# Two buffers each for K and V of a head pair, with their loads requested one job ahead, in a fused attention and two-MLP kernel

## The reference

```python
# q, k, v: (2 batches, 8 heads, 768 positions, 64)
k_sum = k.reshape(B, H, nb, block, D).max(axis=3)       # block 32, nb 24
v_sum = v.reshape(B, H, nb, block, D).mean(axis=3)
scores_l = scale * q @ k.T          # kept where |i - j| < 16, else -1e9
scores_s = scale * q @ k_sum.T + log(block)
a = softmax(concat(scores_l, scores_s)); out = a @ concat(v, v_sum)
x = out as (1536 tokens, 512)
h = relu(x @ w_in);  x = (h * h) @ w_out                 # 512 -> 2048 -> 512
h = x @ w2_in;  solu = h * softmax(h)                    # 512 -> 1024
out = (layer_norm(solu) * g_ln) @ w2_out                 # 1024 -> 512
```

## Time and profile before

| | |
|---|---|
| median of three runs | 531.06 us (530.66 to 531.28) |
| span of the profiled execution | 529.4 us (no separate time was kept for it) |
| TensorE matmul busy | 492.2 us, 93% of the span |
| TensorE weight loads busy | 436.5 us, 82% |
| VectorE busy | 268.0 us, 51% |
| ScalarE busy | 223.8 us, 42% |
| GpSimd busy | 36.2 us, 7% |
| read from and written to HBM | 40.08 MB and 9.44 MB |
| mean granted TensorE clock | 0.970 |

### The profile page before, as it was taken

One profiled execution on the slowest core, in us unless ns is written; L12 is line 12 of the kernel. 1 busy time (PEld: TensorE's weight loads), 2 busy tenths in 40 slices (PEclk: granted clock), 3 DMA queues, 4 the chain that ended last, 5 costly groups with the idle time before them and its releaser, 6 DMA issues.

```text
span 529.4 us, 8722 instructions
## 1 busy us (share of the span) xinstructions
PE 492.2 (93%) x3088; PEld 436.5 (82%) x3088; DVE 268.0 (51%) x548; ACT 223.8 (42%) x553; POOL 36.2 (7%) x45
## 2 busy tenths in 40 slices
PE   3346699999999999999999999999999999999997
PEld 2235499999989999989999999999987888888875
DVE  5456276576575455564644454355374444444330
ACT  3345366556464444453443443333243233333331
POOL 0005411211100000000000000000010000000000
PEclk9966599999999999999999999999999999999999
DMA  7367453342450311232210034222062112211011
GB/s 228 114 207 273 140 156 87 120 140 79 138 181 36 95 36 64 87 133 93 79 40 1 1 104 165 69 61 59 21 195 64 60 62 79 78 60 59 22 39 40
DMA packets 29783, 49.82 MB, mean 94 GB/s; under 512 B 2272, under 2 KB 16864, under 8 KB 29248
## 3 DMA queue, kind: packets, MB, share of 16 engines
q1 hardware_dynamic: 23424, 30.65, 18.9%
q10 hardware_dynamic: 4608, 8.39, 5.4%
q0 software_dynamic: 1728, 10.49, 5.3%
HBM read 40.08 MB, written 9.44 MB: 94 GB/s over the span
## 4 chain that ended last, share of the span: by engine, by line
PE 91%; issue 4%; DVE 2%; DMA 1%; ACT 0%; SPq 0%; ACTq 0%
PE bank L790 27%; PE bank L765 26%; PE bank L896 13%; PE bank L917 13%; PE bank L726 5%; PE bank L746 3%; PE bank L735 2%; PE bank L908 2%; DMA v_raw<-vT 1%; DMA q_sb<-qT 0%; DVE k_ext L535 0%; PE bank L754 0%; DVE k_sum L540 0%; DVE neg_max L557 0%; DVE probs L553 0%
## 5 line engine op out<-in xcount | busy, mean ns | idle before, releaser
L790 PE MATMUL bank<-h_hi,wout_hi 128*128 128x384 f32 x256 | 91.1, 356 | 0.4 <-DVE h_lo L610 0.4
L765 PE MATMUL bank<-x_hi,win_hi 128*128 (+1 forms) x256 | 90.2, 352 | 0.8 <-DVE x_lo L574 0.8
L765 PE MATMUL bank<-x_hi,win_lo 128*128 (+1 forms) x256 | 86.9, 339 | 0.0
L765 PE MATMUL bank<-x_lo,win_hi 128*128 (+1 forms) x256 | 86.8, 339 | 0.0
L790 PE MATMUL bank<-h_hi,wout_lo 128*128 128x384 f32 x256 | 86.4, 337 | 0.0
L790 PE MATMUL bank<-h_lo,wout_hi 128*128 128x384 f32 x256 | 86.1, 336 | 0.0
L409 ACT ACTIVATE relu<-bank 128x384 f32<-128x384 f32 x64 | 31.4, 490 | 103.4 <-PE bank L765 101.4
L607 DVE TENSOR_TENSOR relu<-relu 128x384 f32<-128x384 f32 x64 | 35.7, 558 | 64.9 <-ACT h_hi L414 64.9
L355 ACT ACTIVATE probs<-probs,neg_max 128x118 f32<-128x118 f32 x96 | 36.8, 384 | 42.7 <-DVE neg_max L557 42.7
L790 PEld LDWEIGHTS bank<-h_hi,wout_hi 128*128 128x128 f32 x256 | 48.0, 188 | 5.1 <-issue 3.9
L726 PE MATMUL bank<-k_ext,q_sb 64*64 64x118 f32 x384 | 31.4, 304 | 21.8 <-issue 16.1
(11 more groups left out here) (66 smaller groups left out, 776.7 us busy)
## 6 DMA issues: line engine op xcount, KB each, us to landing
wstage<-wtiles ACTq DMA_DIRECT2D x32, 256.0 KB, 2.7
k_raw<-kT SPq DMA_DIRECT2D x16, 399.0 KB, 3.1
v_raw<-vT SPq DMA_DIRECT2D x16, 384.0 KB, 3.4
v_ext<-vwin SPq DMA_DIRECT2D x16, 282.0 KB
w_in_raw<-w_in_c POOLq DMA_DIRECT2D x4, 1024.0 KB, 6.8
q_sb<-qT SPq DMA_DIRECT2D x16, 192.0 KB, 9.3
y_dram<-x_hi POOLq DMA_DIRECT2D x4, 768.0 KB, 3.8
y_dram<-x_lo POOLq DMA_DIRECT2D x4, 768.0 KB, 4.7
```

The source lines that it names most:

```text
L765: last = nc.tensor.matmul(bank[:, 6 + f % 2, 0:CH], win[a][:, f * WC + k * P:f * WC + (k + 1) * P], rhs, start=(k == 0 and a == 0 and b == ...
L790: last = nc.tensor.matmul(bank[:, 2 + d, 0:CH], wout[a][:, f * WC + d * P:f * WC + (d + 1) * P], h[b][:, f % 2, :], start=(f == 0 and a == ...
```

## The change

`k_raw` and `v_raw` get a second slot, and `k_in` and `v_in` become two semaphores each, one for each slot. A job's K and V go to slot g % 2. The start now requests K and V of job 0 and of job 1; `job(g)` requests K and V of job g + 2, in the same places and behind the same waits where it requested those of job g + 1; the last two jobs request none. GpSimd's wait for K of job 4 is now a wait for the third K of slot 0. Core of the diff (in `windows_k` and `sums_v` only the slot and the wait's value are new):

```diff
-        k_raw = sb(att, "k_raw", [P, S + QT], F32)
-        v_raw = sb(att, "v_raw", [P, S], F32)
+        k_raw = sb(att, "k_raw", [P, 2, S + QT], F32)
+        v_raw = sb(att, "v_raw", [P, 2, S], F32)
...
-                after = at(i, g0 + 1, 2) % PPB + (at(i, g0 + 1, 2) // (2 * PPB)) * PPB
+                after = at(i, g0 + 2, 2) % PPB + (at(i, g0 + 2, 2) // (2 * PPB)) * PPB
...
                     sp.wait_ge(ksum_ok, at(i, g0 + 1, 2))
-                    load_k(after)
+                    load_k(after, slot)
                     sp.wait_ge(vsum_ok, at(i, g0 + 1, 2))
-                    load_v(after)
+                    load_v(after, slot)
...
-            load_k(0)
+            load_k(0, 0)
             load_q(0, 0)
             sp.dma_start(mask[:, 0:UC], mask_c[:, 0:UC]).then_inc(mask_in, 16)
-            load_v(0)
+            load_v(0, 0)
+            load_k(1, 1)
             sp.dma_start(ident[:, :], ident_c).then_inc(const_in, 16)
+            load_v(1, 1)
             sp.dma_start(mask[:, UC:], mask_c[:, UC:]).then_inc(mask2_in, 16)
             sp.dma_start(g_sb[:, :], g_cols).then_inc(const_in, 16)
...
-            job(JOBS - 2, 0)
+            job(JOBS - 2, 0, more=False)
...
-            pool.wait_ge(k_in, 16 * 5)
+            pool.wait_ge(k_in[0], 16 * 3)
...
-                dve.wait_ge(k_in, g * 16 + 16)
+                dve.wait_ge(k_in[slot], arrived)
...
-                dve.wait_ge(v_in, g * 16 + 16)
+                dve.wait_ge(v_in[slot], arrived)
```

More of the change, by code:

```diff
@@ L133, in build @@
         q_in = [sem(f"q_in{i}") for i in range(2)]
-        k_in, v_in = sem("k_in"), sem("v_in")
+        k_in = [sem(f"k_in{i}") for i in range(2)]
+        v_in = [sem(f"v_in{i}") for i in range(2)]
         vw_in = [sem(f"vw_in{i}") for i in range(2)]
@@ L215, in _, with load_k, load_v @@
         def _(sp):
[L216 to L221, removed]
+            def load_k(g, slot):
+                sp.dma_start(k_raw[:, slot, 0:S + 2 * MARGIN],
+                             kT[bass.ds(g, 1), :, :].rearrange("a p s -> (a p) s")).then_inc(k_in[slot], 16)
+            def load_v(g, slot):
+                sp.dma_start(v_raw[:, slot, :],
+                             vT[bass.ds(g, 1), :, :].rearrange("a p s -> (a p) s")).then_inc(v_in[slot], 16)
             def load_q(g, slot):
@@ L530, in _, with windows_k, sums_v @@
         def _(dve):
-            def windows_k(g, slot, half):
+            def windows_k(g, slot, half, arrived):
                 dst = k_ext[:, slot, :].rearrange("p (t c) -> p t c", t=TPJ)
-                dve.wait_ge(k_in, g * 16 + 16)
+                dve.wait_ge(k_in[slot], arrived)
                 nc.vector.tensor_copy(dst[:, :, NB:NB + QT],
-                                      k_raw[:, bass.ds(half * CH, CH)].rearrange("p (t c) -> p t c", t=TPJ))
+                                      k_raw[:, slot, bass.ds(half * CH, CH)].rearrange("p (t c) -> p t c", t=TPJ))
                 nc.vector.tensor_copy(dst[:, :, NB + QT:KX],
-                                      k_raw[:, bass.ds(half * CH + QT, CH)].rearrange("p (t c) -> p t c", t=TPJ)
+                                      k_raw[:, slot, bass.ds(half * CH + QT, CH)].rearrange("p (t c) -> p t c", t=TPJ)
                                       [:, :, 0:WIN - QT])
                 nc.vector.tensor_reduce(k_sum[:, slot, :],
-                                        k_raw[:, MARGIN:MARGIN + S].rearrange("p (n b) -> p n b", b=BLOCK),
+                                        k_raw[:, slot, MARGIN:MARGIN + S].rearrange("p (n b) -> p n b", b=BLOCK),
                                         AX.X, ALU.max).then_inc(ksum_ok, 1)
-            def sums_v(g, slot):
-                dve.wait_ge(v_in, g * 16 + 16)
-                nc.vector.tensor_reduce(v_sum[:, slot, :], v_raw[:, :].rearrange("p (n b) -> p n b", b=BLOCK),
+            def sums_v(g, slot, arrived):
+                dve.wait_ge(v_in[slot], arrived)
+                nc.vector.tensor_reduce(v_sum[:, slot, :], v_raw[:, slot, :].rearrange("p (n b) -> p n b", b=BLOCK),
                                         AX.X, ALU.add).then_inc(vsum_ok, 1)
@@ L575, in x_low @@
                                         x_hi[:, chunk % 2, cols].bitcast(F32), ALU.subtract).then_inc(xlo_ok, 1)
-            windows_k(0, 0, 0)
-            sums_v(0, 0)
+            windows_k(0, 0, 0, 16)
+            sums_v(0, 0, 16)
             for s in range(UPC + 4):
@@ L594, in _ @@
                     if s % UPJ == 0:
-                        windows_k(g, g % 2, g // PPB)
+                        windows_k(g, g % 2, g // PPB, 16 * (g // 2 + 1))
                     else:
-                        sums_v(g, g % 2)
+                        sums_v(g, g % 2, 16 * (g // 2 + 1))
             dve.wait_ge(xlo_ok, UPC)
@@ L630, in body @@
                         more = not (last and e == 1)
+                        arrived = at(i, 16 * (((c + 1) * PPB + e + 1) // 2 + 1), 16)
                         def w_out_low(f, z):
@@ L646, in body @@
                                 if r == 0 and more:
-                                    windows_k(g, 1 - e, (g // PPB) % 2)
+                                    windows_k(g, 1 - e, (g // PPB) % 2, arrived)
                             else:
@@ L650, in body @@
                                 if r == 0 and more:
-                                    sums_v(g, 1 - e)
+                                    sums_v(g, 1 - e, arrived)
                 if c < NCHUNK - 2:
```

## The result

The changed kernel takes 533.48 us (median of 19 runs, 531.85 to 535.25) against 531.58 us before (median of 19, 530.66 to 533.70). The ratio, which goes by the means of the 19 runs (533.41 and 531.85), is 1.0029, with a 95% interval of 1.0018 to 1.0039: slower by 1.0 to 2.1 us. Forecast were 532.6 us and +1.5 us. The size came out. Of the reasons, one was right but too large, and one was missing; that the two errors cancelled was luck.

What follows compares the result with a forecast made beforehand. Two DMA engines carrying the 94-row windows were taken to bound the first phase. Removed waits 0, later q of job 1 +1.4 and clock +0.1 gave +1.5 on 531.06: 532.6 us, range 531.0 to 534.3.

Steps and rivals of the forecast that it cites:

- The bound: First 62.5 us: two DMA engines carrying the 94-row windows of V set the pace, not K and not V.
- What the change removes: VectorE's remaining K wait, about 0.1 us, and GpSimd's 0.5 us before the third weight quarter: taken as 0.
- What it moves: At the start, the extra K and V delay q of job 1: 2.4 less 0.96 us absorbed, +1.4, ends 1.0 and 2.8.
- Whether it reaches the end: Gaps up to 57.4 us: each link starts from the one before, so the whole 1.4 us is handed on.
- The constants: Rest of mask and `g_sb` land 2.2 to 2.8 us later, TensorE's second scores at about 11.2; cost nothing.
- The clock: TensorE at 1.2 GHz after the last gap, 57.4 to 64.5 us: +0.1 us, ends -1.0 and +1.0.
- Rival (a): First wait grows by 2.8 us, nothing absorbed, and the clock rises late, +0.7: 534.6 us; chance 0.16.
- (b): Not slower: idle engine time at 8 to 10.6 us absorbs more, clock rises sooner: 531.1 us; chance 0.24, shared.
- (c): Prefetch pays: extra pair hidden, removed waits count in full, -0.6: 530.5 us, or 529.9 with clock; chance 0.08.
- (d): K and V arrive earlier but nobody waits for them: 531.1 us; chance 0.24, shared.

Runs made afterwards that it cites:

- run 10: Kernel before, with GpSimd requesting the third quarter of the weights only after the low parts of the first four weight tiles; 533.82 us, 1.0035.
- run 6: Kernel before, with the third quarter of the weights requested after K of job 3 instead of K of job 4; 532.76 us, 1.0022.
- run 5: Changed kernel, with GpSimd waiting for K of job 5 instead of job 4 before requesting the third quarter of the weights; 532.36 us, 1.0020.
- run 7: Changed kernel, with windows and q requested first for jobs 0 to 2 and the third quarter of the weights requested late; 531.70 us, 0.9997.
- run 2: Changed kernel, with requests for jobs 0 to 2 reordered so that windows of V and q come first; 532.39 us, 1.0014.
- run 1: Kernel before, plus one K and one V of job 1 loaded at the start into spare buffers nobody reads; 532.4 us, 1.0011.
- run 9: Kernel before, plus an unread K and V pair at the start and the third quarter of the weights requested after K of job 3; 533.07 us, 1.0020.
- run 4: Kernel before, with each load of windows of V cut in two, of 80 and 14 rows; 514.28 us, 0.9672.
- run 3: Changed kernel, with each load of windows of V cut in two, of 80 and 14 rows; 514.86 us, 0.9684.
- 11: Kernel before, with windows loads split into 80 and 14 rows and the third quarter of the weights requested late; 520.49 us, 0.9794.
- 12: Changed kernel, with windows and q requested first, windows loads split and the third quarter of the weights requested late; 521.46 us, 0.9798.

## Why the prediction came out

**The bound** (two engines' line of windows): right, and shown. Splitting the loads took q of job 1 from 9.9 to 3.3 us and the kernel from 531.5 to 514.3.

**What the change removes**: the K wait of 0.1 us gave nothing, right. For GpSimd's 0.5 us I took 0, with ends of 0 and a *gain* of 0.5. **This is the step that failed.** The wait did go, and it cost time: the windows of job 3 are waited for longer when the third quarter is asked for earlier, and shorter when it is late (run 10). Four timed pairs differ in the third quarter's request alone: before to run 6, +0.22% of the time; run 5 to the changed kernel, +0.09%; run 7 to run 2, +0.17%; run 1 to run 9, +0.09%. The mean is 0.14%, about 0.8 us; from the intervals of the single ratios I estimate 0.3 to 1.2 us for it. Only the first of them is clear by itself. In the profiles the windows of job 3 held TensorE for 13.3 to 14.7 us with the late request (before, runs 1, 5, 7) and 14.7 to 15.7 with the early one (after, runs 2, 6, 9), 1.1 us more on average. I had written that these engines are "already 0.95 busy" there, and drew from it that nothing could be gained. I did not ask what could be lost: on full engines a load that comes earlier can take its share from the one that is waited for.

**What it moves**: the right mechanism, a term too large. I priced the pair at 2.4 us less 0.96 absorbed, +1.4. The engines carried it at 392 GB/s, above both of my rates, which is 2.0 us for 0.80 MB; less the same 0.96 gives 1.1. The first gap ends at 19.76, 19.21, 19.19 and 19.02 us with the pair (after, runs 1, 5, 9), at 18.82, 18.07 and 18.83 without it (before, runs 6, 10): 0.7 us on average. The first of my ends, +1.0, was nearer.

**Whether it reaches the end**: only in part. In the changed kernel's profile the 0.94 arrives as 1.04 and 0.98 at the next two links, as forecast. But over the four profiles with the pair (after, runs 1, 5, 9) and the three without (before, runs 6, 10), whose requests otherwise are the same up to there, the shift is 0.7 us at the first link, 0.7 at the second and 0.4 at the third. And the three without it, 0.8 us apart at the second link, are within 0.1 at the third. So the links do not simply start one from the other, as the prediction says; what else holds the third one is not shown. In time, run 1 gives +0.11% with an interval that holds zero, and run 5, with the slots too, a clear +0.20%. That the pair costs something is supported by run 5; by run 1 it is between nothing and 1.4 us.

**The constants**: `g_sb` and TensorE's second scores moved as forecast (the scores from 8.69 to 11.12 us, against "about 11.2"), covered by the first gap. **The clock**: +0.1 was taken, and the profiled execution lost some 1.7 us to it, which the median shows little of. It also makes single profiles poor witnesses for tenths of a microsecond. As a rival it does not tell early from late third quarter: TensorE's work at 1.2 GHz after the last restart was 6.3, 9.3, 6.9 and 7.7 us with the late request (before, runs 1, 5, 7) and 9.7, 6.6, 7.0 and 7.4 with the early one (after, runs 2, 6, 9), 0.1 us apart on average. Whether the pair makes the clock rise later stays open: the two highest, 9.3 and 9.7, have it, 6.9 and 7.4 too.

So +1.5 us came from 1.4 + 0.1 in the forecast. In the runs about 0.8 of it goes with the third quarter's place, a term at 0 in the forecast, and the 0.7 that is left with what else run 5 has: the pair, and perhaps the slots. A term too large by as much as another was too small is luck. Rival (a), 534.6 us, had the larger shift and the late clock of the profiled run, but from a pair that is not absorbed at all; rivals (b) and (c) fell with the interval of the ratio. (d) holds in its first half: K and V come earlier and nobody waits for them.

What stays open: why the third link swallows a part of the shift, how the 0.7 us divides, and whether the slots themselves cost a tenth of a percent (after against run 9: 1.0029 to 1.0020, overlapping).

## What to carry to other kernels

Before loads are doubled, look for who waits for them; here nobody did, and the loads only joined the queue of those who are waited for. When an edit removes a wait on the way to a large transfer, ask what that transfer will meet earlier, even if the wait looks like pure loss; when an edit puts a transfer off, ask what work piles up behind it. And a load whose busy share reads 0.13 of 16 engines is worth more than all of it: cutting its 94 rows into 80 and 14 saved 17 us.

## What the runs showed of the hardware

A load of 94 rows kept 0.13 of the 16 engines busy, which is two, at 49 and 50 GB/s together; as 80 and 14 rows it no longer held q up (3.3 us in run 4, 5.0 in run 3). The Trainium skill (DMA: Bandwidth & Descriptors, Why a DMA increments its semaphore by 16 and not by 1) states that the number of engines is the largest divisor up to 16 of the rows; the row of 0.13 busy agrees, since that is 2 for 94. How many engines the two parts ran on, no view here shows.

The burst at the start ran at 289 GB/s, and with one more K and V in it at 325, 392 in its later part: my rate from the smaller burst was too low for the larger one.

Half a microsecond in one request of 1 MB showed in the time of a kernel of 531 us, by 0.22% in run 6 (0.10 to 0.35%).

VectorE's square of a 128x384 tile, 0.56 us by the median of run 10, took 5.1 to 5.7 us in runs 10, 11 and 12, each time until just after the end of five GpSimd instructions in a row. The two VectorE instructions before it in run 10, which began in the same row at 60.33 and 60.89 us, kept their usual 0.53 and 0.52.
